# A gated linear-attention stage on TensorE: scores per head on 64 array rows, decay and mask as two wide products, the exponential's column bias and the division on ScalarE

## What is computed

```python
m_new = np.maximum(f_gate[:, :, t] + m, i_gate[:, :, t])
f_stab = np.exp(f_gate[:, :, t] + m - m_new)
i_stab = np.exp(i_gate[:, :, t] - m_new)
C = f_stab * C + i_stab * outer(vt, kt);  n = f_stab * n + i_stab * kt
y[:, :, t] = sigmoid(o_gate) * (C @ qt) / np.maximum(np.abs(n @ qt), 1.0)
```

## Time and profile before

| | us |
|---|---|
| median of 3 runs | 872.5 |
| lowest, highest | 869.71, 875.26 |
| the profiled execution's own time | 880.63 |
| span of its instructions | 878.9 |

### The profile page before, as it was taken

One profiled execution on the slowest core, in us unless ns is written; L12 is line 12 of the kernel. 1 busy time (PEld: TensorE's weight loads), 2 busy tenths in 40 slices (PEclk: granted clock), 3 DMA queues, 4 the chain that ended last, 5 costly groups with the idle time before them and its releaser, 6 DMA issues. The chain is left out here.

```text
span 878.9 us, 17001 instructions
## 1 busy us (share of the span) xinstructions
PE 729.0 (83%) x5044; PEld 672.5 (77%) x5044; DVE 529.1 (60%) x1622; ACT 290.1 (33%) x756; POOL 413.2 (47%) x557
## 2 busy tenths in 40 slices
PE   0999999994328795986959799983899998999897
PEld 0899999993217684866847698982899997999896
DVE  6479999985775556555556545445546364464462
ACT  4222222220014241422314246451524254245241
POOL 6568878871043452352426375874224043242341
PEclk9999999996558897897779799996899998999999
DMA  8857666625431411223221424535462424623610
GB/s 272 190 148 191 193 186 187 179 79 171 115 130 29 145 48 45 91 87 95 87 73 50 132 66 140 180 105 161 158 206 73 145 70 116 201 81 124 186 33 17
DMA packets 99641, 109.59 MB, mean 125 GB/s; under 512 B 39053, under 2 KB 83726, under 8 KB 99568
## 3 DMA queue, kind: packets, MB, share of 16 engines
q1 hardware_dynamic: 85792, 74.83, 29.8%
q10 hardware_dynamic: 9696, 21.24, 7.5%
q0 software_dynamic: 4080, 12.61, 4.5%
HBM read 89.45 MB, written 20.02 MB: 125 GB/s over the span
## 5 line engine op out<-in xcount | busy, mean ns | idle before, releaser
L535 POOL TENSOR_TENSOR parts_w2l<-all_w,parts_w2h 128x320 fp32r<-128x320 f32 x128 | 113.5, 903 | 131.2 <-ACT parts_w2h L522 128.2
L595 DVE SCALAR_TENSOR_TENSOR l_hl<-bank,l_hh 128x384 fp32r<-128x384 f32 (+1 forms) x168 | 83.1, 494 | 137.6 <-ACT l_hh L591 134.9
L591 ACT ACTIVATE l_hh<-bank 128x384 fp32r<-128x384 f32 (+1 forms) x168 | 74.0, 440 | 167.5 <-PE bank L576 163.0
L572 PE MATMUL bank<-l_xh,parts_w1h 128*128 128x384 f32 x256 | 94.8, 370 | 23.1 <-DVE l_xh L565 12.6
L573 PE MATMUL bank<-l_xl,parts_w1h 128*128 128x384 f32 x256 | 90.0, 352 | 0.0
L574 PE MATMUL bank<-l_xh,parts_w1l 128*128 128x384 f32 x256 | 89.8, 351 | 0.0
L529 POOL TENSOR_TENSOR parts_w1l<-all_w,parts_w1h 128x384 fp32r<-128x384 f32 x72 | 70.3, 1005 | 38.8 <-ACT parts_w1h L515 38.8
L1343 PE MATMUL bank<-parts_w2h,l_hh 128*128 128x320 f32 x192 | 74.4, 387 | 7.1 <-issue 7.1
L582 PE MATMUL bank<-parts_w2h,l_hh 128*128 128x320 f32 x232 | 74.5, 321 | 0.0
L572 PEld LDWEIGHTS bank<-l_xh,parts_w1h 128*128 128x128 f32 x256 | 50.9, 199 | 29.1 <-issue 15.2
L584 PE MATMUL bank<-parts_w2h,l_hl 128*128 128x320 f32 x232 | 71.6, 309 | 0.0
(11 more groups left out here) (253 smaller groups left out, 1900.5 us busy)
## 6 DMA issues: line engine op xcount, KB each, us to landing
all_w<-in_moe_w SPq DMA_DIRECT2D x10, 1280.0 KB, 6.3
all_w<-in_moe_w SPq DMA_DIRECT2D x10, 1024.0 KB
all_w<-in_moe_w ACTq DMA_DIRECT2D x6, 1280.0 KB, 12.5
att_kT<-in_kT SPq DMA_DIRECT2D x24, 256.0 KB, 2.8
att_qD<-in_qT SPq DMA_DIRECT2D x48, 128.0 KB, 3.1
att_qT<-in_qT SPq DMA_DIRECT2D x24, 256.0 KB, 3.1
all_w<-in_moe_w ACTq DMA_DIRECT2D x6, 1024.0 KB
all_w<-in_moe_w SPq DMA_DIRECT2D x20, 256.0 KB
```

The lines of the kernel that those rows point to most:

```text
L535: ops.tensor_tensor(sh.w2l[:, r, p, :], sh.w2[:, p, :], sh.w2h[:, r, p, :].bitcast(FP), ALU.subtract).then_inc(sh.w2_low, 1)
L572: T.matmul(dst, sh.w1h[:, r, k, f], xh[:, k, :], start=k == 0, stop=False)
L591: return nc.scalar.activation(hh, src, ACT.Relu)
L595: return nc.vector.scalar_tensor_tensor(hl, src, 0.0, hh.bitcast(FP), ALU.max, ALU.subtract)
```

## The change

Scores: four fp32 products of 128 columns on 64 array rows each, head j of a pair into bank j of a pair of banks; `qD`, its loads and its zeroing go. Decay: one bank instead of two; the product of an identity with the mask (128 rows, 512 columns, bf16) starts a sum, to which a product of three rows (ones with `G_flat`, 512 columns, bf16) is added. `G_flat` holds the three bf16 parts of G on one partition each; three DMAs make it from `G_parts`. ScalarE then makes the exponential per head out of PSUM with colT as bias, and the scaling by rden per head. `log_weights` and `col_mask` go. The transposes of a token tile come one step later and ahead of `outputs`. The gate terms are made on 32 partitions by DVE alone, and an exponential of one column ahead of the loop loads the table.

```diff
-QLOADS = 5
+QLOADS = 3
-        gate = sb("gate", [3 * BH, 2, S])
+        gate = sb("gate", [BH, 2, S])
...
+        G_parts, G_flat = sb("G_parts", [BH, 3, S], BF), sb("G_flat", [3, BH, S], BF)
+        mask, eye = sb("mask", [P, P], BF), sb("eye", [P, P], BF)
...
-        p_G, p_S, p_O, p_L = bank[1:3], bank[3:5], bank[5:7], bank[7]
+        p_G, p_O, p_L = bank[0], bank[5:7], bank[7]
+        p_S = [sh.psum[:, 1 + 2 * i:3 + 2 * i, 0:PR * P] for i in range(2)]
...
             tile_load(0, 0, True)
             sp.dma_start(wg[:, :, :, :].rearrange("p g j e -> p (g j e)"), a["w_gates"]).then_inc(in_wg, 16)
+            for i in range(3):
+                sp.wait_ge(parts_done, i + 1)
+                sp.dma_start(G_flat[i:i + 1, :, :], G_parts[:, i, :]).then_inc(flat_in[i], 16)
             for b in range(1, B):
                 tile_load(0, b, True)
...
             def weights(c, k):
-                wait_done(act, D_done, u)
-                nc.scalar.activation(eGl[:, k % QB, :], p_G[k % 2][:, :].rearrange("p (h t) -> p h t", t=P)[:, :, P - 1],
-                                     ACT.Exp).then_inc(eGl_done, 1)
-                nc.scalar.activation(w, w, ACT.Exp).then_inc(W_done, 1)
+                wait_done(act, P_done, u - QB)
+                wait_done(act, wv_done, u - QB)
+                wait_done(act, G_psum, u)
+                nc.scalar.activation(eGl[:, k % QB, :], p_G[:, :].rearrange("p (h t) -> p h t", t=P)[:, :, P - 1],
+                                     ACT.Exp).then_inc(eGl_done, 1)
+                for h in range(HU):
+                    x = nc.scalar.activation(W[:, k % QB, h, :], p_G[:, h * P:(h + 1) * P], ACT.Exp,
+                                             bias=colT[:, bass.ds(c * BH + (k * HU + h), 1)])
+                x.then_inc(W_done, 1)
...
+            def scale(c, k):
+                wait_done(act, rd_done, u)
+                wait_done(act, y_done, u - 2)
+                for h in range(HU):
+                    x = nc.scalar.activation(scaled[:, k % 2, h, :], num[:, ring, h, 0:D], ACT.Copy, scale=rden[:, ring, h:h + 1])
+                x.then_inc(scaled_done, 1)
...
             def decay_rows(c, k):
-                wait_done(pe, D_done, u - 2)
-                wait_done(pe, eGl_done, u - 2)
+                wait_done(pe, W_done, u - 1)
-                for h in range(HU):
-                    mm = nc.tensor.matmul(p_G[k % 2][:, h * P:(h + 1) * P], pick_row[:, bh:bh + 1].to_broadcast([3 * BH, P]),
-                                          G_parts[:, bass.ts(c, P)], start=True, stop=True)
+                every = p_G[:, :].rearrange("p (h t) -> p h t", t=P)
+                nc.tensor.matmul(every, eye[:, :], mask[:, :].unsqueeze(1).to_broadcast([P, HU, P]), start=True, stop=False)
+                nc.tensor.matmul(every, sh.ones_b[0:3, :], G_flat[:, k * HU:(k + 1) * HU, bass.ts(c, P)],
+                                 start=False, stop=True).then_inc(G_psum, 1)
...
                 for r in range(PR):
-                    mm = nc.tensor.matmul(p_S[par][:, 2 * r * P:(2 * r + 2) * P], kT[:, b, pair, :],
-                                          qD[:, b, pair, :, :].rearrange("p j t -> p (j t)"), start=True, stop=True)
+                    for j in range(2):
+                        rows = slice(PW * j, PW * (j + 1))
+                        mm = nc.tensor.matmul(p_S[par][:, j, r * P:(r + 1) * P], kT[rows, b, pair, :], qT[rows, b, pair, :],
+                                              start=True, stop=True)
...
                 if k >= 0:
+                    if k % 2:
+                        x_transposes(c, k)
                     outputs(c, k)
-                    if k % 2 == 0:
-                        x_transposes(c, k)
-                    else:
+                    if k % 2:
                         logits(c, k - 1)
```

More of the change, by code:

```diff
@@ L84, in attention @@
         X = sb("X", [P, NT + 1, DM])
-        bands = [slice(i * BH, (i + 1) * BH) for i in range(3)]
-        gate = sb("gate", [3 * BH, 2, S])
+        gate = sb("gate", [BH, 2, S])
         ig, fg = gate[:, 0, :], gate[:, 1, :]
[L89 to L93, removed]
+        m, lf, G, col, rm = (sb(x, [BH, S]) for x in ("m", "lf", "G", "col", "rm"))
+        rest = [lf, rm]
+        G_parts, G_flat = sb("G_parts", [BH, 3, S], BF), sb("G_flat", [3, BH, S], BF)
+        mask, eye = sb("mask", [P, P], BF), sb("eye", [P, P], BF)
+        warm = sb("warm", [P, 1])
         eG, colT = sb("eG", [P, NC * BH]), sb("colT", [P, NC * BH])
         qT, kT = (sb(x, [P, B, PB, P]) for x in ("qT", "kT"))
-        qD = sb("qD", [P, B, PB, 2, P])
         k_ = sb("k", [P, B, DM])
@@ L116, in attention @@
         in_o = [sem(f"in_o{c}") for c in range(NC)]
-        gate_o, zeroed = sem("gate_o"), sem("zeroed")
+        gate_o, warmed, flat_in = sem("gate_o"), sem("warmed"), [sem(f"flat_in{i}") for i in range(3)]
         G_psum, S_psum, O_psum, xT_psum, L_psum = pe_sems = [
             sem(x) for x in ("G_psum", "S_psum", "O_psum", "xT_psum", "L_psum")]
[L120 to L124, removed]
+        eGl_done, W_done, xT_done, scaled_done = act_sems = [sem(x) for x in ("eGl_done", "W_done", "xT_done", "scaled_done")]
+        P_done, inter_done, num_done, den_done, rd_done, C_done, L_done = dve_sems = [
+            sem(x) for x in ("P_done", "inter_done", "num_done", "den_done", "rd_done", "C_done", "L_done")]
+        wv_done, Cd_done, y_done = pool_sems = [sem(x) for x in ("wv_done", "Cd_done", "y_done")]
         X_in = [sem(f"X_in{b}") for b in range(B)]
@@ L177, in _ @@
             nc.gpsimd.memset(rm[:, :], 1.0).then_inc(pg, 1)
-            nc.gpsimd.memset(mask[:, :], 0.0).then_inc(pg, 1)
-            pool.wait_ge(pg, 2)
+            pool.wait_ge(pg, 1)
             nc.gpsimd.memset(rm[:, :].rearrange("p (c t) -> p c t", t=P)[:, :, 0:1], 0.0).then_inc(consts, 1)
             pool.wait_ge(consts, 1)
-            for j in range(2):
-                nc.gpsimd.memset(qD[PW * (1 - j):PW * (2 - j), :, :, j, :], 0.0).then_inc(zeroed, 1)
-                pool.wait_ge(zeroed, j + 1)
+            nc.gpsimd.memset(warm[:, :], 0.0).then_inc(pg, 1)
             nc.gpsimd.memset(C[:, :, :, :], 0.0).then_inc(consts, 1)
@@ L188, in _ @@
             nc.gpsimd.memset(xs[:, B - 1, :], 0.0).then_inc(consts, 1)
-            nc.gpsimd.affine_select(out=mask[:, :], in_=mask[:, :], pattern=[[1, P]], compare_op=ALU.is_ge,
[L191 to L213, removed]
+            nc.gpsimd.memset(num[:, QB - 1, :, :], 0.0).then_inc(consts, 1)
+            nc.gpsimd.memset(rden[:, QB - 1, :], 0.0).then_inc(consts, 1)
+            nc.gpsimd.memset(mask[:, :], 0.0).then_inc(pg, 1)
+            nc.gpsimd.tensor_copy(eye[:, :], ident[:, :]).then_inc(consts, 1)
+            pool.wait_ge(pg, 3)
+            nc.gpsimd.affine_select(out=mask[:, :], in_=mask[:, :], pattern=[[1, P]], compare_op=ALU.is_ge,
+                                    fill=NEG, base=0, channel_multiplier=-1).then_inc(consts, 1)
+            pool.wait_ge(consts, 8)
             def weighted_values(c, k):
@@ L247, in step @@
             def step(c, k, last):
-                if not (last and k + 3 >= UPC):
-                    col_mask(c, k + 3)
                 if not (last and k + 2 >= UPC):
@@ L284, in step @@
                     weights(c, k + 2)
-                if k >= 0 and k % 2 == 0:
-                    copy_xT(c, k)
+                if k >= 0:
+                    if k % 2:
+                        copy_xT(c, k)
+                    scale(c, k - 1)
             for c in range(NC):
@@ L295, in _ @@
                     nc.scalar.activation(x, x, ACT.Sigmoid).then_inc(gate_o, 1)
+            act.wait_ge(pg, 2)
+            nc.scalar.activation(warm[:, :], warm[:, :], ACT.Exp).then_inc(warmed, 1)
             act.wait_ge(colT_done, 1)
-            act.wait_ge(consts, 4)
+            act.wait_ge(consts, 8)
             nc.scalar.activation(eG[:, :], p_L[:, NC * BH:2 * NC * BH], ACT.Exp).then_inc(eG_done, 1)
             steps(act, step)
-            copy_xT(NC - 1, UPC)
+            scale(NC - 1, UPC - 1)
+            copy_xT(NC - 1, UPC + 1)
+            act.wait_ge(warmed, 1)
         @block.vector
@@ L322, in _ @@
             for i in range(2):
-                nc.vector.tensor_copy(part[:, :], left[:, :]).then_inc(dg, 1)
-                dve.wait_ge(dg, 7 + i)
-                nc.vector.tensor_tensor(rest[i][:, :], left[:, :], part[:, :], ALU.subtract).then_inc(rest_done, 1)
+                nc.vector.tensor_copy(G_parts[:, i, :], left[:, :]).then_inc(parts_done, 1)
+                dve.wait_ge(parts_done, i + 1)
+                nc.vector.tensor_tensor(rest[i][:, :], left[:, :], G_parts[:, i, :], ALU.subtract).then_inc(rest_done, 1)
                 dve.wait_ge(rest_done, i + 1)
                 left = rest[i]
+            nc.vector.tensor_copy(G_parts[:, 2, :], left[:, :]).then_inc(parts_done, 1)
+            nc.vector.tensor_tensor(col[:, :], ig, m[:, :], ALU.subtract).then_inc(dg, 1)
```

(10 more changed lines are left out.)

55 lines of the change are left out of this document (18 added, 37 removed).

## The result

The changed kernel takes 1016.37 us (median of 4 runs, 1015.94 to 1020.01), the one before 873.88 beside it. The forecast was 1007.5, between 981 and 1034.

What follows compares the result with a forecast made beforehand. PE was taken to bound the attention stage. Low-clock units and the stage's end, +135.6, four units ahead, +0.5, and the start, -1, made +135 us on the 872.5 us median: 1007.5 us, between 981 and 1034.

Steps and rivals of the forecast that it cites:

- The bound: Attention stage: PE sets the pace, listed busy 147.15 of 147.80 us; DVE follows at 90%.
- The clock: Attention stage: PE stays at 1.2 GHz nearly throughout, 6.50 us a unit instead of 3.50; chance 0.54.
- three breaks: Each unit's PE stream: three new form changes, between 128, 3, 64 and 128 rows, interrupt the wide products.
- The sum: Whole stage: 43 units and the end +135.6, four units ahead +0.5, start -1, together +135 us.
- Decay 0.84 us: Decay products on PE: two of 512 columns take 0.84 us at the low clock, for 0.42 before.
- Scores side by side: Score products on PE: both array halves work at once, 0.90 us a unit at the low clock, otherwise 1.79.
- The form changes: Between PE's decay and score products: three a unit, each 0.20 us at the low clock, 0.10 at the high.
- its dear end: PE's form changes: each costs twice as much because wide products drain too; 7.10 us a unit, 1034 us in all.
- ScalarE: Exponentials, scalings and copies on ACT: 2.3 us a unit, hidden behind PE at the low clock.
- the 50% named as a sign: VectorE in the stage: busy near 50% would show the forecast right.
- The start: Ahead of PE's first decay product: gate terms and new DMAs change it by -1 us, between -2 and +3.
- the added wait: Decay with one bank: waiting for the exponentials of the unit before costs 0.

Runs made afterwards that it cites:

- e3: The changed kernel with each unit's identity product made five times instead of once: 940.96 us.
- e2: The kernel before with only the halved scores (four products of 128 columns on 64 rows) and one decay bank: 993.29 us, ratio 1.1294.
- e12: e6 with a product of three rows and 8 columns between the two wide decay products, and one added wait: 1025.21 us.
- e6: The changed kernel with the product of ones and G_flat over 128 rows, 125 of them zeros: 900.39 us, ratio 1.0286.
- e10: e6 with wide products on PE ahead of the loop and eight in each of its two lead-in steps: 886.23 us, ratio 1.0172.
- e11: The changed kernel with scores back over 128 rows (two products of 256 columns) and the ones product on 128 rows: 886.45 us, ratio 1.0164.
- e9: The changed kernel with the product of ones and G_flat over 32 rows, 29 of them zeros: 1016.71 us.

## Why the prediction was right

**The bound.** PE's pace sets the stage: right, and e3 says it again, where more PE work at the higher clock took less time.

**The clock.** The largest term: right. The argument (a thinner run of wide products, three breaks) named the right causes: e2 shows that the scores part is enough by itself on the kernel before, e3 that more wide products bring the level back, e12 that the breaks are enough where e6's stream gets it. It was a judgement at 0.54, and the runs show how near the edge it is: e6 and e12 differ by one product of eight columns and lie 125 us apart.

**The sum.** +135 us was forecast for the stage and 133.9 measured, but that closeness is in part luck, since its pieces erred in both directions. From the scores of the fifth unit to those of the last, 43 units, it is 276.9 us for 150.4, +126.5 (+129 forecast: 6.44 us a unit instead of 6.50). The stretch ahead of it takes 2.8 us more (0.5 less forecast), the end 4.6 more (6.6 forecast).

**The terms per unit.** Decay 0.84 us: right (wide products in a row start 0.43 us apart in e3's low stretch). Scores side by side: right; the eight records start in four pairs, the two of a pair 6 to 7 ns apart. The Trainium skill, TensorE: Matmul & The Clock Gate, Part 3, has products in different row groups overlap, some 4 ns apart; the trace agrees with the overlap. The form changes were put at 0.20 each at the low clock: the two in front of and behind the ones product took 151.10 - 150.55 = 0.55 and 151.63 - 151.10 = 0.53 us for 0.43 of streaming, 0.11 each on average. Scores to what follows took 1.15 for 0.86, 0.29 more, about half of it between the first pair and the second (0.37 us apart, the others 0.21). In all 0.51 for 0.60, and 2.23 us for 2.34. The step from 0.10 at the high clock to 0.20 at the low one isn't borne out: at the high clock e6 has 122.20 - 121.89 = 0.31 us for 0.21 of streaming, 0.10, as much as at the low one. The Trainium skill, TensorEngine Tiling (Array Packing), Key Properties, says that a change of mode drains TensorE, which the prediction took for its dear end, 0.40 a change; none of the three places measured that much. Whether the array drains there, the rows can't tell.

**ScalarE.** One exponential is listed at 0.37 us and one scaling at 0.33, for 0.27 and 0.19 in the sum. But they overlap, and it is the group of four that counts: 1.14 us (1.06 forecast) and 0.99 (0.74).

```profile
159.31 1.14 ACT L245 ACTIVATE att_W<-banks,att_colT 128x128 f32<-128x128 f32 x4
160.32 0.99 ACT L263 ACTIVATE att_scaled<-att_num,att_rden 128x40 f32<-128x40 f32 x4
```

From 47 to 195 us ScalarE is busy for 55.54 of 147.80 us, 2.4 us a unit for 2.3. PE covered it at both levels (e10, e11). VectorE is busy for 36% of that stretch, not near the 50% named as a sign: 133.09 us for 42 units before less 0.69 each would be 2.5 us a unit of 6.5, 38%.

**The start.** -1 us was forecast. PE's first product is at 23.79 us as before, but now behind the new DMAs; and the first scores start at 27.43 us, before at 24.59, 2.8 us later. With one bank the second unit's decay waits for the exponentials of the first, 1.47 us (and the third's 0.31). The sum put the added wait at nothing; that holds in the loop and fails once, in the lead-in. The kernel after, and the first scores of the kernel before:

```profile
23.79 0.59 PE L403 MATMUL banks<-att_mask,att_eye 128*128 128x512 bf16 x1 [5.51 <-DMA att_G_flat<-att_G_parts]
...
26.38 0.59 PE L403 MATMUL banks<-att_mask,att_eye 128*128 128x512 bf16 x1 [1.47 <-ACT att_W L245]
...
27.43 1.22 PE L417 MATMUL banks<-att_qT,att_kT 64*128 64x128 f32 x8
```
```profile
24.59 2.02 PE L435 MATMUL bank<-att_qD,att_kT 128*128 128x256 f32 x4
```

**What wasn't in the sum.** The part from the first weight product of the experts on took 617.0 us in this trace and 611.4 before. In the experiments it is between 609.3 and 617.8 with the same code. So of the nine us by which the forecast was low, 5.6 lie there and -1.1 in the stage. The other 4.5 come from the medians: the profiled execution before was 8.1 us above the median that the forecast started from, the one after 3.6 above its own.

## What to carry to other kernels

Packing small products onto parts of the array can save PE's work and cost its clock (e2: 0.51 us less work a unit, 2.5 us more time): before halving the stream of an engine that sets the pace, look at the durations of the same instruction in stretches at both levels and ask which of them the new stream will resemble. Order products by the number of rows they use, so that the form changes as seldom as can be. Where the trace has no record of the clock, judge it by the durations of the same instruction, and never by "busy".

## What the runs showed of the hardware

Two changes of form for an 8-column product kept a stage of 48 units at 1.2 GHz that without them rose to 2.4 GHz behind its eighth unit (e12 and e6). A three-row product is worth no more and no less than a 32-row one in this stream (e9: 1016.71 us, and 1016.37). A change of form from 128 rows to three and back cost PE about 0.11 us each at 1.2 GHz (the kernel after). Three DMAs of 48 KB, each from 32 partitions to one, took 8.6 to 11.2 us to land beside the other loads of the start:

```profile
DMA to landing us min/median/max: 8.6/9.9/11.2
```
